# A two-layer kernel gets three written-out orders of work (beginning, middle, end), block-wise first convolutions, one fixed PSUM bank for layer 1 and extra buffers for the last tiles

## The reference

```python
w = softmax(weight, axis=-1)                    # 8 heads x 7 taps, one head per 24 channels
x = causal_conv(x, w)                           # 7 taps along the sequence, per channel -> (8192, 192)
h = x @ moe_w_in                                # 192 -> 2048
x = (h * np.clip(h + 3.0, 0.0, 6.0) / 6.0) @ moe_w_out          # -> (8192, 192)
h = x @ moe2_w_in
P = a[0] + a[1] * h + a[2] * h**2 + a[3] * h**3
Q = 1.0 + np.abs(b[0]) * np.abs(h) + np.abs(b[1]) * h**2
out = (P / (Q + 1e-06)) @ moe2_w_out
```

## Time and profile before

| | us |
|---|---|
| median of 3 runs | 1254.16 (1252.77 to 1256.11) |
| the profiled execution | 1255.71 |
| its span, first to last instruction | 1253.9 |
| TensorE busy | 1194.4 |
| VectorE busy | 1170.2 |
| ScalarE busy | 1168.9 |
| GpSimd busy | 1080.4 |
| mean granted TensorE clock | 0.988 |

### The profile page before, as it was taken

How to read it: one execution, slowest core, us unless ns; L and a number is a source line. 1 busy time by engine, 2 the same in 40 slices (tenths; PEclk the granted TensorE clock), 3 DMA queues, 4 the chain that set the end, 5 groups by cost and what they waited for, 6 DMA issues and landing times.

```text
span 1253.9 us, 18222 instructions
## 1 busy us (share of the span) xinstructions
PE 1194.4 (95%) x5120; PEld 963.1 (77%) x5120; DVE 1170.2 (93%) x1784; ACT 1168.9 (93%) x2223; POOL 1080.4 (86%) x828
## 2 busy tenths in 40 slices
PE   4989999999999999999999999999999999999766
PEld 3767778888788888888788887888878887888554
DVE  6779999999999999999999999999999999998797
ACT  4779999999999999999999999999999999999896
POOL 3759898998989899998989989998999989888565
PEclk8999999999999999999999999999999999999899
DMA  4310000000000000010000100000000000000000
GB/s 123 125 39 10 1 22 1 17 14 1 22 1 22 10 7 16 1 31 1 22 1 1 30 1 23 1 22 10 1 22 1 22 1 14 1 1 13 1 14 13
DMA packets 10005, 21.17 MB, mean 17 GB/s; under 512 B 1712, under 2 KB 1712, under 8 KB 9904
## 3 DMA queue, kind: packets, MB, share of 16 engines
q1 hardware_dynamic: 9760, 19.55, 5.3%
q10 hardware_dynamic: 144, 0.46, 0.1%
HBM read 13.72 MB, written 6.29 MB: 16 GB/s over the span
## 4 chain that ended last, share of the span: by engine, by line
PE 79%; DVE 11%; issue 5%; ACT 5%; POOL 0%; DMA 0%; SPq 0%; ACTq 0%; DVEq 0%; POOLq 0%
PE h L236 39%; PE y0b_acc L253 4%; PE y0a_acc L248 4%; PE y0b_acc L254 4%; PE y0a_acc L250 4%; PE y0a_acc L249 4%; PE y1a_acc L248 4%; PE y1b_acc L254 4%; PE y1a_acc L249 4%; PE y1b_acc L253 4%; PE y1a_acc L250 4%; DVE num L365 2%; DVE h L397 2%; DVE g L404 1%; ACT h L387 1%
## 5 line engine op out<-in xcount | busy, mean ns | idle before, releaser
L377 POOL TENSOR_TENSOR den<-den,sqr 128x512 f32<-128x512 f32 x256 | 377.4, 1474 | 124.7 <-ACT den L354 123.8
L415 POOL TENSOR_TENSOR g_lo<-g,g_hi 128x512 fp32r<-128x512 f32 x256 | 336.2, 1313 | 1.9 <-ACT g_hi L421 1.9
L341 POOL TENSOR_TENSOR g_lo<-r,g_hi 128x512 fp32r<-128x512 f32 x234 | 307.5, 1314 | 0.0
L370 DVE SCALAR_TENSOR_TENSOR num<-num,coef,h 128x512 f32<-128x512 f32 x256 | 191.5, 748 | 9.1
L397 DVE SCALAR_TENSOR_TENSOR h<-num,coef,h 128x512 f32<-128x512 f32 x256 | 191.8, 749 | 0.0
L392 DVE SCALAR_TENSOR_TENSOR den<-den,h 128x512 f32<-128x512 f32 x256 | 174.5, 682 | 17.5 <-ACT h L387 15.3
L381 ACT ACTIVATE rsq<-den 128x512 f32<-128x512 f32 x256 | 165.3, 646 | 25.8 <-POOL den L377 24.9
L365 DVE TENSOR_TENSOR num<-num,h 128x512 f32<-128x512 f32 x256 | 175.1, 684 | 12.4 <-ACT num L348 4.8
L348 ACT ACTIVATE num<-h,coef 128x512 f32<-128x512 f32 x256 | 182.2, 712 | 0.0
L404 DVE SCALAR_TENSOR_TENSOR g<-den,h 128x512 f32<-128x512 f32 x256 | 174.3, 681 | 0.7
L421 ACT ACTIVATE g_hi<-g 128x512 fp32r<-128x512 f32 x256 | 168.7, 659 | 3.2 <-DVE g L404 1.6
(11 more groups left out here) (93 smaller groups left out, 2886.6 us busy)
## 6 DMA issues: line engine op xcount, KB each, us to landing
stage_w<-w_pack SPq DMA_DIRECT2D x15, 448.0 KB, 3.3
raw_a<-x_a SPq DMA_DIRECT2D x16, 259.0 KB, 3.4
out<-y_a SPq DMA_DIRECT2D x16, 256.0 KB, 2.7
raw_b<-x_b SPq DMA_DIRECT2D x16, 129.5 KB, 2.7
out<-y_b SPq DMA_DIRECT2D x16, 128.0 KB, 2.4
stage_w<-w_pack ACTq DMA_DIRECT2D x1, 448.0 KB, 3.5
tap_a<-taps SPq DMA_DIRECT2D x1, 3.5 KB, 2.9
tap_b<-taps SPq DMA_DIRECT2D x1, 3.5 KB, 4.0
```

The costliest lines, as they stand in the source:

```text
L341: eng.tensor_tensor(g1_lo[q.off % 2][:, :], gated(q)[:, :], f32(g1_hi[q.off % 2][:, :]), ALU.subtract).then_inc(S["g1lo"], 1)
L370: eng.scalar_tensor_tensor(out=n, in0=n, scalar=a1, in1=h2_of(q), op0=ALU.add, op1=ALU.mult).then_inc(S["num1"], 1)
L377: eng.tensor_tensor(d, d, sqr[q.off % 2][:, :], ALU.add).then_inc(S["den_sum"], 1)
L415: eng.tensor_tensor(g2_lo[q.off % 2][:, :], g2[q.off % 2][:, :], f32(g2_hi[q.off % 2][:, :]), ALU.subtract).then_inc(S["g2lo"], 1)
```

## The change

- The steps become a list, `course`. Layer 2 starts at step 20 instead of 21, and after step 233 one extra step belongs to layer 2 alone, so layer 2 has 19 tiles left after the last layer-1 tile's step instead of 21.
- There are three plans. `BEGIN` (layer 1 alone) gives `out1` a lag of 3 and issues `g1hi` and `g1lo` one step after `relu1` and `gate1`. `MIDDLE` has the same lags as before with a changed order inside a step. `END` (from step 258) is an order of its own, without layer-1 tiles.
- The weight work is cut into four stages, each issued by a pace of 1.35 steps per chunk, and all of it except the rounding is on GpSimd.
- In the setup the taps come in one transfer. The convolution of block 0 sums in layer 1's idle accumulators in PSUM. The b part of blocks 0 and 1 is convolved one block at a time, 256 columns over 128 partitions, with the two halves of the columns on the two halves of the partitions; its split then takes two instructions of 64 x 256 each.
- Layer 1 keeps one hidden bank from tile 20 on, without swaps; layer 2 goes round three, and four after layer 1's last tile.
- From layer-2 tile 240 on, the reciprocal goes to layer 1's accumulators (`quotient`), so `rec2` no longer waits for `num1`, the hidden bank is free after `num1` and `abs2`, and the denominator has four buffers. For the very last tile `den_sum` and `g2lo` are on VectorE.
- The two output transfers of a block have a semaphore each.

The core of the diff (helpers that only lose the `Step` class are left out):

```diff
-BANK_SWAP = (7, 15, 23, 31)
...
-IN1, IN2, OUT1, OUT2 = 0, 21, 2, 25
-EARLY = 22
-SUM1, SUM2 = 16 + OUT1, 16 + OUT2
+IN2, OUT1 = 20, 2
+EARLY = IN2 + 1
+SPARE = 240
+EXTRA = (233,)
+SUM1, SUM2 = 16 + OUT1, 20
 AHEAD, PAIR_AHEAD = -16, -32
 
 
-SCHEDULE = {
-    "tensor": [("in1", IN1), ("in2", IN2), ("out1", OUT1), ("out2", OUT2)],
-    "scalar": [("x2b_hi", SUM1, 0), ("cs_b_hi", AHEAD, 13, 0), ("y2a_out", SUM2, 0),
-               ("y1a_out", SUM1, 0), ("x2a_hi", SUM1, 1), ("y2b_move", SUM2, 0), ("rsq2", 22),
-               ("relu1", 0), ("conv_b_first", PAIR_AHEAD, 11, 0), ("cs_b_hi", AHEAD, 3, 1), ("rec2", 22),
-               ("conv_a_first", AHEAD, 1), ("sq2", 21), ("abs2", 21), ("cs_a_hi", AHEAD, 10),
-               ("lin2", 21), ("g1hi", 0), ("g2hi", 23)],
-    "vector": [("g1lo_early", 1), ("num2", 22), ("cs_b_lo", AHEAD, 14, 0), ("num1", 22),
-               ("x2b_res", SUM1, 0), ("cs_b_lo", AHEAD, 10, 1), ("x2b_lo", SUM1, 0), ("g_neg", 23),
-               ("y2b_sum", SUM2, 0), ("gate1", 0), ("newton", 22), ("conv_a", AHEAD, (1, 4, 5, 6, 7, 8)),
-               ("conv_b_head", PAIR_AHEAD, (11, 12, 13), 0), ("conv_b_tail", AHEAD, (10, 11, 12), 0),
-               ("g_first", 22)],
-    "gpsimd": [("den_sum", 21), ("cs_a_lo", AHEAD, 10), ("g1lo", 0), ("g2lo", 23), ("x2a_lo", SUM1, 0)],
+BEGIN = {
+    "sync": [("load_a", AHEAD, 0), ("load_b", PAIR_AHEAD, 9, 0), ("load_w", -4)],
+    "tensor": [("in1", 0), ("out1", 3)],
+    "scalar": [("relu1", 0), ("y1a_out", SUM1, 0), ("x2b_hi", SUM1, 0), ("conv_b_first", PAIR_AHEAD, 13, 0),
+             ("g1hi", 1), ("cs_b_hi", AHEAD, 16, 0), ("w_in_hi", 0), ("x2a_hi", SUM1, 0), ("w_out_hi", 1),
+             ("cs_a_hi", AHEAD, 10), ("conv_a_first", AHEAD, 1), ("cs_b_hi", AHEAD, 9, 1)],
+    "vector": [("cs_b_lo", AHEAD, 10, 1), ("gate1", 0), ("x2b_res", SUM1, 0),
+             ("conv_b1", AHEAD, (2, 3, 5, 5, 5, 7, 8), 1), ("conv_b_tail", AHEAD, (10, 10, 12), 0), ("g1lo", 1),
+             ("conv_b_head", PAIR_AHEAD, (12, 12, 13), 0), ("x2b_lo", SUM1, 0), ("cs_b_lo", AHEAD, 13, 0),
+             ("conv_a", AHEAD, (1, 4, 5, 6, 8, 9))],
+    "gpsimd": [("cs_a_lo", AHEAD, 10), ("w_in_lo", 0), ("w_out_lo", 0), ("x2a_lo", SUM1, -2)],
 }
-LATE = ["sq2", "den_sum", "num2", "in2", "y2b_move", "num1", "y2b_sum", "out2", "y2a_out", "rsq2",
-        "rec2", "g_neg", "abs2", "newton", "g_first", "g2lo", "lin2", "g2hi"]
...
+MIDDLE = {
+    "sync": [("load_a", AHEAD, 0), ("load_b", PAIR_AHEAD, 0, 0), ("store_y", SUM2, 1)],
+    "tensor": [("in1", 0), ("in2", 0), ("out1", 2), ("out2", 4)],
+    "scalar": [("y2b_move", SUM2, 0), ("y2a_out", SUM2, 0), ("x2b_hi", SUM1, 0), ("cs_b_hi", AHEAD, 13, 0),
+             ("conv_a_first", AHEAD, -1), ("y1a_out", SUM1, 0), ("rsq2", 1), ("relu1", 0), ("x2a_hi", SUM1, 0),
+             ("rec2", 1), ("conv_b_first", PAIR_AHEAD, 11, 0), ("sq2", 0), ("abs2", 0),
+             ("cs_b_hi", AHEAD, 5, 1), ("lin2", 0), ("cs_a_hi", AHEAD, 10), ("g1hi", 0), ("g2hi", 2)],
+    "vector": [("num2", 1), ("num1", 1), ("g1lo", 2), ("cs_b_lo", AHEAD, 15, 0), ("x2b_res", SUM1, 0),
+             ("x2b_lo", SUM1, 0), ("y2b_sum", SUM2, 0), ("g_neg", 2), ("gate1", 0), ("newton", 1),
+             ("cs_b_lo", AHEAD, 10, 1), ("conv_a", AHEAD, (1, 4, 5, 6, 7, 8)),
+             ("conv_b_head", PAIR_AHEAD, (11, 13, 14), 0), ("conv_b_tail", AHEAD, (10, 11, 12), 0),
+             ("g_first", 1)],
+    "gpsimd": [("x2a_lo", SUM1, 0), ("den_sum", 0), ("g1lo", 0), ("g2lo", 2), ("cs_a_lo", AHEAD, 13)],
+}
+END = {
+    "sync": [("store_y", SUM2, 1)],
+    "tensor": [("in2", 0), ("out2", 4)],
+    "scalar": [("x2b_hi", SUM1, 0), ("y1a_out", SUM1, 0), ("sq2", 0), ("rsq2", 1), ("x2a_hi", SUM1, 0),
+             ("y2a_out", SUM2, -1), ("rec2", 1), ("abs2", 0), ("lin2", 0), ("g2hi", 2), ("y2b_move", SUM2, -2)],
+    "vector": [("num2", 1), ("x2b_res", SUM1, 0), ("g2lo", 4), ("num1", 1), ("g_neg", 2), ("y2b_sum", SUM2, -1),
+             ("x2b_lo", SUM1, 0), ("newton", 1), ("den_sum", 0), ("g_first", 1)],
+    "gpsimd": [("x2a_lo", SUM1, 0), ("den_sum", 0), ("g2lo", 2)],
+}
+W_PACE = 1.35
+END_AT = 258
...
-    turn1, turn2, free = [], [], list(range(H_BANKS))
-    for p in range(STEPS):
-        own = free.pop()
-        oldest = free.pop(0)
-        if p in BANK_SWAP:
-            own, oldest = oldest, own
-        turn1.append(own)
-        turn2.append(oldest)
-        free += [oldest, own]
-    assert free == list(range(H_BANKS))
...
+    course, p, s = [], -1, -1
+    while s < NT + SUM2 - NF + 1:
+        one = p < NT + SUM1 - NF + 1
+        p += one
+        two = p >= IN2
+        s += two
+        course.append((p, s, one, two))
+        if one and p in EXTRA:
+            s += 1
+            course.append((p, s, False, True))
+    bank1, bank2, bank_free, user = {}, {}, {}, {}
+    def take(layer, tile, own):
+        bank_free[layer, tile] = user.get(own, ())
+        if layer == 0:
+            user[own] = (("gate1", tile + 1),)
+        elif tile < SPARE:
+            user[own] = (("g_done", tile + 1),)
+        else:
+            user[own] = (("num1", tile + 1), ("abs2", tile + 1))
+    kept = (IN2 - 1) % H_BANKS
+    turn = [(kept + 1 + i) % H_BANKS for i in range(H_BANKS - 1)]
+    for p, s, one, two in course:
+        if one and p < NT:
+            bank1[p] = p % H_BANKS if p < IN2 else kept
+            take(0, p, bank1[p])
+        if two and s < NT:
+            if p >= NT and kept not in turn:
+                turn.insert(0, kept)
+            bank2[s] = turn[0]
+            turn.append(turn.pop(0))
+            take(1, s, bank2[s])
...
+        def quotient(t):
+            return ([ya_acc[0], yb_acc[0]][t % 2] if t >= SPARE else h_banks[bank2[t]])[:, :]
+        def den_of(t):
+            return ((den + r1)[t % 4] if t >= SPARE else den[t % 2])[:, :]
...
+        def wait_bank(eng, layer, t):
+            for name, count in bank_free[layer, t]:
+                eng.wait_ge(S[name], count)
...
+        def abs2(eng, t):
+            eng.wait_ge(S["h2_done"], t + 1)
+            if t < SPARE + 2:
+                after(eng, S["g_done"], t - 1)
+            elif t < SPARE + 4:
+                eng.wait_ge(S["g1lo"], NT)
+            else:
+                eng.wait_ge(S["g_done"], t - 3)
+            eng.activation(den_of(t), h2_of(t), ACT.Abs, scale=reg_b0).then_inc(S["abs2"], 1)
...
+        def den_sum(eng, t):
+            if (t == NT - 1) != (eng is nc.vector):
+                return
+            eng.wait_ge(S["abs2"], t + 1)
+            eng.wait_ge(S["sq2"], t + 1)
+            if t == NT - 1:
+                eng.wait_ge(S["den_sum"], t)
+            eng.tensor_tensor(den_of(t), den_of(t), sqr[t % 2][:, :], ALU.add).then_inc(S["den_sum"], 1)
...
+        def rec2(eng, t):
+            eng.wait_ge(S["rsq_done"], t + 1)
+            if t < SPARE:
+                eng.wait_ge(S["num1"], t + 1)
+            elif t < SPARE + 2:
+                eng.wait_ge(S["y1a_out"], NB)
+                eng.wait_ge(S["x2b_lo"], NB)
+            else:
+                eng.wait_ge(S["g_done"], t - 1)
+            eng.activation(quotient(t), rsq[t % 2][:, :], ACT.Square).then_inc(S["rec"], 1)
...
+        def g_first(eng, t):
+            eng.wait_ge(S["rec"], t + 1)
+            if t >= SPARE:
+                eng.wait_ge(S["num1"], t + 1)
+            eng.scalar_tensor_tensor(out=quotient(t), in0=num[t % 2][:, :], scalar=a0, in1=quotient(t),
...
+        def sums_a(k):
+            return (conv_a if k else ya_acc[0])[:, :]
+        def sums_b(k):
+            return conv_b[:, :] if k > 1 else [yb_acc[0], conv_b][k][:, 0:HALF]
+        def taps_b(k):
+            return K * k if k < 2 else K * (k // 2 + 1)
...
         def conv_b_tap(eng, k, j):
-            own, w = S["conv_b_tap"], tap[1][:, j:j + 1]
+            w, acc = tap[1][:, j:j + 1], sums_b(k)
+            at, n = (k * HW, HALF) if k < 2 else (0, BLK)
             if j == 0:
-                wait_count(eng, d_raw_b, pair(k).times(2 * 16), 2 * 16)
-                wait_count(eng, S["cs_b_lo"], k, 0)
-                scaled(eng, conv_b[:, :], raw_b[:, 0:BLK], w).then_inc(own, 1)
+                eng.wait_ge(d_raw_b, 32 * (k + 1 if k < 2 else k // 2 + 2))
+                after(eng, S["cs_b_lo"], k)
+                ins = scaled(eng, acc, raw_b[:, at:at + n], w)
             else:
-                wait_taps(eng, own, pair(k), j)
-                eng.scalar_tensor_tensor(out=conv_b[:, :], in0=raw_b[:, j:j + BLK], scalar=w,
-                                         in1=conv_b[:, :], op0=ALU.mult, op1=ALU.add).then_inc(own, 1)
+                eng.wait_ge(S["conv_b_tap"], taps_b(k) + j)
+                ins = eng.scalar_tensor_tensor(out=acc, in0=raw_b[:, at + j:at + j + n], scalar=w,
+                                               in1=acc, op0=ALU.mult, op1=ALU.add)
+            ins.then_inc(S["conv_b_tap"], 1)
...
+        def places(k):
+            lower, upper = slice(0, DB), slice(DB, P)
+            if k < 2:
```

(78 more changed lines are left out.)

520 lines of the change are left out of this document (207 added, 313 removed).

## The result

The changed kernel takes 1225.17 us (median of 4 runs, 1224.98 to 1226.22), the one before 1253.97 beside it: ratio 0.977, 95% interval 0.9753 to 0.9787. That is 28.8 us less; the forecast was 1228, with 1218 to 1239. The profiled execution of the changed kernel took 1226.22, of which 1224.4 is the span: 29.5 less than before, where the sum had 26.3.

What follows compares the result with a forecast made beforehand. Shares named no single bound; TensorE loses 94.2 us to waits and low clock, mostly at beginning and end. Terms: -15.2 + 4.6 - 3 + 3.4 - 16.1 = -26.3, off the median 1254.16: 1228, range 1218 to 1239 (own range 1223 to 1233).

Steps and rivals of the forecast that it cites:

- the end's step of 3.25: Layer-2 tail: with `rec2` waiting for `rsq2` alone, a step takes 3.25 us instead of 3.46.
- the price of the half taps: Setup, VectorE: a tap of 256 columns takes 0.52 us, so seven b taps take 2.0 us less.
- the middle's step: Steps of both layers: expected near 4.58 us; a change of 0.02 or more would make the prediction wrong.
- a tile of layer 1 alone: Beginning: TensorE paces a tile at 2.27 us; over 2.4 would make the prediction wrong.
- no excess: Setup, VectorE's a taps: with the sum in PSUM, no added time beside GpSimd; 0.4 us earlier.
- rival A: Beginning: weight conversions or taps beside GpSimd keep a tile at 2.6, in1(20) at 69, total 1233.5; chance 0.17.
- the 63.5 of the forecast: Beginning: in1(20) starts at 63.5 instead of in1(21) at 78.70, -15.2 us; bounds 61.5 and 69.
- the gap ahead of the b pass: Setup: TensorE's 4.17 us idle shrinks to 1.5; whether 2.4 GHz holds is open, at worst 2 us, half hidden.
- I take -3: Middle: moved entries can take away or add small waits, 14.4 us in all; -3 us, bounds -10 and +5.
- rival C: Middle: the recurring waits nearly all go, -11 us instead of -3, total 1220; chance 0.14.
- Rival D: Middle: one bank for layer 1 makes `in1` wait for `gate1` in every step, total 1281; chance 0.04.
- Rival B: End: late starts add up to today's step, the tail gives 8 us instead of 16, total 1236; chance 0.17.

Runs made afterwards that it cites:

- b_sbuf: Changed kernel with the sums of the first two convolutions in SBUF instead of the idle accumulators, halves kept: 1230.27 us, ratio 0.9792.
- m_swap: Changed kernel with layer 1 and layer 2 exchanging hidden banks at every eighth step again: 1224.94 us, ratio 0.9773.
- m_pool: Changed kernel with only GpSimd's list in the middle plan in its former order (`den_sum` first, `x2a_lo` last): 1238.12 us, ratio 0.987.
- m_csb: Changed kernel with `cs_b_lo` of the odd blocks ahead of `gate1` on VectorE again in the middle plan: 1228.53 us, ratio 0.9798.
- m_csalo: Changed kernel with only `cs_a_lo` on GpSimd three steps earlier again, `x2a_lo` still first: 1228.26 us, ratio 0.9785.
- m_old: Changed kernel with the `MIDDLE` lists of ScalarE, VectorE and GpSimd in their former order, all else as changed: 1240.46 us, ratio 0.989.
- t_midend: Changed kernel with `MIDDLE`'s order kept to the end; the last tile's `den_sum` and `g2lo` added to VectorE's list: 1230.49 us, ratio 0.9813.
- t_noextra: Changed kernel without the extra step of layer 2 after step 233: 1225.77 us, ratio 0.9772.
- t_recwait: Changed kernel with `rec2` waiting for `num1` again in the last 16 tiles: 1227.58 us, ratio 0.9787.

## Why the prediction was right, and where it was off

The forecast of 1228 and its own range of 1223 to 1233 hold the 1225.2, and the end's step of 3.25, the fixed bank and the price of the half taps came as the mechanism said. But two of the signs under which the prediction called itself wrong did appear: the middle's step changed by 0.045 us (147.01 and 145.56 over 32), more than its 0.02, and a tile of layer 1 alone takes 2.46 on the mean, more than its 2.4. That the total is only 3.2 off is in part luck, for the misses have opposite signs.

**Setup.** The b pass came at 17.65 against 18.1, 3.5 earlier than before and not 3. The half taps cost 3.12 / 6 = 0.52, as worked out from the two widths of the earlier trace rows, and seven of them 2.1 less than before. The Trainium skill (VectorE: DVE Perf Modes, section "The TRN2 errata — SBUF-src ops pay a fixed extra latency per instruction") gives 58 cycles for an operation from SBUF to SBUF, by which the prediction estimated 0.33; the sum here is in PSUM, and for a source in PSUM the same table has 120, by the same estimate 0.39. The trace, with 0.52, bears out neither. The first taps cost 5.47 together, 0.11 less than before and not 0.4; but here "no excess" meant more than the term said, for GpSimd now works beside them (b_sbuf, 4.0 us). Between the last a tap and the first b tap, where `w_lo_in` stood, 1.3 is gone instead of 0.7, the split adds 0.4 instead of 0.25, and 0.4 has no term at all: the first tap starts at 5.35 instead of 5.77.

**Layer 1 alone.** From in1(4) to in1(19) eleven of the fifteen tiles take 2.27, as forecast, and TensorE paces them. The other four take 2.71, 2.72, 3.13 and 3.32; the first of them holds a low clock, the others a late `g1lo`. The worst:

```profile
49.48 2.71 DVE L543 SCALAR_TENSOR_TENSOR conv_b<-raw_b,tap_ab,conv_b 128x512 f32<-128x512 f32 x2 [0.88 <-ACT conv_b L550]
...
52.83 0.60 ACT L445 ACTIVATE g_hi<-y1b_acc 128x512 fp32r<-128x512 f32 x1 [1.73 <-DVE y1b_acc L332]
```

Two taps of 512 columns take 1.3 each beside GpSimd, `gate1` comes behind them, ScalarE idles for 1.73 ahead of `g1hi`, and TensorE for 0.80 ahead of `out1`. The prediction wanted no idle time of ScalarE ahead of `g_hi` in the first 60 us. Ten rows have some; eight of them wait for TensorE, which still reads the `g_hi` before (so TensorE sets the pace there), and two, this one and one of 0.47 at 37.43, for `gate1`. So rival A (taps beside GpSimd, 2.6 a tile, in1(20) at 69) names what happens in these three steps, and is wrong about the others.

In1(20) came 2.3 us later than the 63.5 of the forecast. The trace has 155 matmuls from `out1` of tile 1 to in1(20), 35.1 us; the forecast had 16 tiles, 36.3, and so counted half a tile, 1.1, too much. `out1` of tile 1 started at 26.26 instead of 24.5, +1.8. The small waits (0.21, 0.60 and 0.80 in the brackets) make their three tiles 2.4 longer, by the distance of starts, and not 0.6: +1.8. The wait for `x2b_lo`, 1.52 in its bracket, costs 1.9 by the distance of starts instead of 1.4: +0.5. `gate1` of tile 19 costs nothing instead of 0.7. That is 1.8 + 1.8 + 0.5 - 0.7 - 1.1 = 2.3. Most of the first item is the clock: in the changed kernel and in m_swap every instruction up to step 20 is the same, `out1` of tile 1 came at 26.26 in the one and at 24.71 in the other, and in1(20) at 65.80 and 64.61. The windows of the changed kernel:

```profile
20.00:30.00 10.00, 7.57 (x27) 6.13 (x28) 8.27 (x14) 8.17 (x17) 7.57 (x8) 0.83 0.26 80
60.00:70.00 10.00, 8.48 (x29) 6.23 (x28) 6.86 (x10) 6.05 (x13) 4.21 (x6) 0.83 0.00 0
```

and of m_swap:

```profile
20.00:30.00 10.00, 7.64 (x33) 6.17 (x34) 9.26 (x15) 9.32 (x19) 8.33 (x10) 1.00 0.28 92
60.00:70.00 10.00, 8.50 (x37) 6.39 (x36) 7.21 (x11) 7.35 (x15) 4.92 (x5) 1.00 0.01 2
```

The column ahead of the last two is the granted clock, as a share of 2.4 GHz. Where it reads 0.83, a stretch ran at 1.2 GHz. The matmuls there start 0.43 us apart:

```profile
67.95 0.63 PE L263 MATMUL h<-x1a_hi,win_lo 128*128 128x512 f32 x1
68.38 0.63 PE L263 MATMUL h<-x1a_lo,win_hi 128*128 128x512 f32 x1
```

In1(32) comes at 122.40 with both low stretches and at 119.62 without, in m_pool at 119.60, also without. The prediction had put this at up to 2 us, half of it hidden, and took nothing for it in the sum; it costs 2.8 when both come. It had looked for it at the gap ahead of the b pass; there, after 1.32 of idle time, the matmuls start 0.23 apart, and the clock falls at the next wait, 2.67 ahead of the first `out1`. The second stretch is missing in the traces of m_csb, m_csalo, m_old and t_midend too. What decides between executions stays open.

**Middle.** Here a term was mis-sized: "I take -3" measured -7.9. From mark to mark the middle takes 1073.56. Taking from it the step that lies between the marks more than before (4.53) and the extra step (2.5 by t_noextra, where the forecast had 3.4) leaves 1066.5 against 1074.4: -7.9 instead of -3. It is made up of the stretch from in1(32) to in1(255), 1016.96 less 2.5 against 1024.62 before, -10.2, and of the fill in front of it, 56.60 less the added step against 49.77 before, +2.3 (in m_swap, without the low clock, 55.01, so 1.6 of it is the clock). The whole lies between the forecast's -3 and rival C's -11, nearer to C. Against C it was said that VectorE and ScalarE are 97% busy there; they still are. What made the difference was the place of GpSimd's and VectorE's block operations in their queues (m_pool, m_csb, and m_old with all three lists), which the prediction had taken to "take away or add waits of this size" without pricing any of them: 147.01 to 145.56 a pair. With the old order the kernel would have taken 1240, and none of the forecast's terms says so, since the extra step and `IN2` = 20 were priced as if `x2a_lo` could be no later than before. The extra step and the order belong together (m_pool); an old order with the old start at step 21 was not run.

The fixed bank is worth nothing beside this order, as forecast (m_swap). Rival D, one bank as a wait in every step, shows nowhere: no `in1` of the steady stretch waits over 0.1 for `gate1`.

**End.** The step of 3.25 is exact. That the whole, 85.0, comes so near to 84.7 is luck, for its terms moved against each other: in2(255) came after 64.3 instead of 68.5, and the rest took 20.7 instead of 16.2. In part the mark misleads: in2(255) stands 7.5 ahead of its tile's `rec2`, before it stood 6.4 ahead, probably since banks come free earlier now (not shown by a run). For a tail that VectorE and ScalarE set, `rec2` is the mark to count by: the last one comes 71.8 after in1(255) instead of 89.3, and the stretch behind it takes 13.2 instead of 11.5. The forecast had made this last stretch shorter, since the last tile's `den_sum` and `g2lo` are on VectorE. `den_sum` there does bring `rec2` forward, but not `newton`, which stands in VectorE's own queue and comes 1.72 behind it (0.63 before):

```profile
1211.15 0.60 ACT L406 ACTIVATE y0b_acc<-rsq 128x512 f32<-128x512 f32 x1
...
1212.87 0.68 DVE L410 SCALAR_TENSOR_TENSOR r<-r,y0b_acc 128x512 f32<-128x512 f32 x1
```

So the traces show no gain for that step; it was not run by itself. Of the 15.8, t_recwait gives 2.5 to the freed `rec2`, t_midend 4.8 to the own order, t_noextra 3.0 to the tile that left the tail; the other 5 or so (one more tile from `IN2` = 20, and the spare banks and buffers) were not taken apart. These shares were each measured with the rest in place, so their sum is rough. Rival B, the last tiles keep today's step, is refuted by the 3.25, though t_midend shows that its mechanism waits behind the order.

**Total.** -12.9 - 0.8 - 15.8 = -29.5 against -26.3: the beginning 2.3 short, the middle 5.8 better (4.9 by the term of -3, 0.9 by the extra step), the end 0.3 short.

## What to carry to other kernels

When a schedule brings two dependent stages closer (an earlier start, an extra step), list every engine's queue between the one that makes the operand and the one that takes it. Where two steps between them were enough for the queue, one step became a stall of the queue's length, here 3.7 us of GpSimd's work. An idle PSUM accumulator is a good place for a running sum of VectorE if GpSimd works at the same time. And a list of small recurring waits is worth pricing one by one, by what stands ahead of the late operation in its queue: 0.045 us a step was 10 us here.

## What the runs showed of the hardware

A half tap of 256 columns takes 490 ns with its sum in PSUM and 755 ns with its sum in SBUF, both in the changed kernel (the groups by form):

```profile
L543 DVE SCALAR_TENSOR_TENSOR conv_b<-raw_b,tap_ab,conv_b 128x256 f32<-128x256 f32 x6 | 4.5, 755 | 0.1
L543 DVE SCALAR_TENSOR_TENSOR y0b_acc<-raw_b,tap_ab,y0b_acc 128x256 f32<-128x256 f32 x6 | 2.9, 490 | 0.2
```

Five of the six in SBUF, and all six in PSUM, run beside GpSimd's work on the weights. The one in SBUF that does not (GpSimd has nothing between 25.32 and 26.61) is as short as those in PSUM:

```profile
25.43 0.48 DVE L543 SCALAR_TENSOR_TENSOR conv_b<-raw_b,tap_ab,conv_b 128x256 f32<-128x256 f32 x1
```

b_sbuf, where nothing but the place of the sum is changed, shows the same from the other side: 3.95 for the six of block 0 in SBUF, 3.12 in PSUM. So a sum in SBUF is slow while GpSimd works, and not by itself. Why, was not tested.

TensorE's clock differs between executions of the same instructions. t_midend is the changed kernel up to in1(255); from in1(20) to in1(32) it takes 54.98, without a low stretch there, where the changed kernel takes 56.60 with one. With the low stretch ahead of in1(20) it comes to some 3 us of this kernel's time (122.40 against 119.62 at in1(32)).
